# Token mix of a Fourier mixer on one core: order of GpSimd's sums, PE's chunk as one loop, first pairs among the last tiles of the MLP stage

## The chip, the cores and the metric

One core of a Trainium2 chip runs the whole program. The metric is the device time of the program in microseconds, lower is better. Several runs of each kernel are timed; one more execution is profiled, and every duration below comes from that one.

## The reference

Three blocks one after the other on x of 4 x 4224 x 192 in float32. The first is a causal convolution over 7 tokens whose weights are a softmax of `weight_gen`; the second adds the real part of a two-dimensional Fourier transform and an MLP. The third is the one that matters here:

```python
theta = x @ w_theta
zr, zi = x * np.cos(theta), x * np.sin(theta)
y = np.einsum('ts,bsd->btd', w_tok_r, zr) + np.einsum('ts,bsd->btd', w_tok_i, zi)
u = x + y
return u + np.maximum(u @ w_ch, 0.0)
```

The two einsums multiply weights of 4224 x 4224 with operands of 4224 x 768. They are the largest part of the work: the token mix.

## The kernel before, in words

**Stages.** A (convolution and the first Fourier pass), B (second Fourier pass), C (MLP, `run_c(step_c, ...)` over tiles n = 0 to 32 of 128 tokens, with the angle theta, its sine and cosine and z = x cos, x sin trailing a tile or two behind), M (token mix) and E (the last chunk of the mix, with the final product with `w_ch` woven in). Each engine has its own program; they meet only at semaphores.

**The token mix.** The tokens that are summed over are split into 11 chunks of three tiles. In each chunk 16 pairs of output tiles are treated, in four rounds `jj` of four pairs `i4` (pair p = 4 jj + i4), and a 33rd tile that is left over. A pair is a two by two block product (two output tiles, real and imaginary operand, two halves of the columns) done with seven products in place of eight, from sums and differences of blocks. A product is nine matmuls of 128x128 by 128x384 (three tiles, and each factor as a high and a low float32r part, without low by low), so a pair is 63 matmuls (`products`, L1448; `product`, L1456).

**Weights.** SP loads four blocks of a pair (`load_pair`, L463) into one of two buffers. GpSimd makes four sums of them (`sum_w`, L989, called by `sums`, L1029, which waits until the low parts of the pair before are made, because the four `wsum` tiles are single). ScalarE rounds each to its high part `wh` (`high_w`, L1154), VectorE subtracts for the low part `wl` (`low_w`, L720). The weights of pair p + 1 are made product by product while TensorE works on pair p.

**Operands.** The high and low parts of z for a chunk, `zh` and `zl`, stand twice, one set by `par`. While chunk c is multiplied, the three tiles of chunk c + 1 are prepared, one in each of the rounds jj = 0, 1, 2: SP loads the tile (`load_z`, L471) in the first pair of the round, GpSimd makes four sums (`sum_z`, L978), ScalarE and VectorE make seven high and low parts at the places of `ZPLACE` (L327): three in the second pair of the round (after products 1, 3 and 5), two in the third (after 2 and 5) and two in the fourth.

**Results.** After each product VectorE adds PSUM to the buffer `rbuf` of the pair (`add_r`, L778). In VectorE's program each `add_r(i)` is followed by `low_w` of the next pair and, where ZPLACE says so, by `low_z`. TensorE's product 2 waits for the add of product 0, product 4 for that of 2, product 6 for that of 4 (L1462 to L1469). So a VectorE instruction that waits holds back the adds that stand behind it, and with them TensorE.

**Loops.** TensorE's chunk (L1499) is a loop over three rounds, then the fourth round written out, then `left_m`. Chunks 1 to 8 are a loop of four passes over two chunks each (L1520). `chunk` of VectorE and ScalarE are built in the same way, as are their loops over two chunks (L860, L1254); the change leaves those loops as they are.

**The passage from C to M.** SP's order at the end of C: three loads of `rbuf`, `step_c` of NT, NT + 1 and NT + 2 (which store the last x2 and z tiles), a wait for all stores, the load of `rl`, and only then its M loop, whose first step loads weights for pair 2 and the z tile 3 (L502 to L536). VectorE reduces the last angles (`reduce_angle`, L710: four instructions on 128x768) between the first pairs' work (L838 to L857), ScalarE takes sines there (L1235 to L1252), GpSimd multiplies z (L1006, L1007) and rounds the turns (L1009, L1011) in its `step_c`. In the last tile of C, ScalarE's copy of theta (L1143) waits for the first instruction of `reduce_angle`, and TensorE's second half of `mlp_down` waits for that copy (L1443).

Of the kernel before, what the change touches and what calls it, by code (L numbers as in the profile page):

```python
# [31 lines left out]
ds = bass.ds  # L32
# [5 lines left out]
NT = S // P  # L38
# [4 lines left out]
NG = NT // 3  # L43
# [62 lines left out]
def token_fourier_mixer(nc, x_pad, wgen, f_seq, f_chan, f_rest, f_low, ident, w1, w2, w_theta, w_pairs, w_left,  # L106
# [15 lines left out]
    with ExitStack() as top:  # L122
# [160 lines left out]
        def live(m):  # L283
            return not isinstance(m, int) or 0 <= m < NT
# [19 lines left out]
        def flat(t):  # L304
            return t[:].rearrange("p b d -> p (b d)")
# [68 lines left out]
        def _(sp):  # L374
# [128 lines left out]
            sp.wait_ge(y_ready, 2 * NT)  # L503
            for k in range(3):
                load_r(k, k)
            for n in range(NT, NT + 3):
                step_c(n, n)
            sp.wait_ge(z_out, 16 * NT)
            sp.wait_ge(y_out, 16 * NT)
            sp.dma_start(flat(rl), y_scr[NT - 1:NT].rearrange("o p x -> p (o x)")).then_inc(rl_in, 16)  # L510


            def step_m(c, jj, i4):

                p = pair(jj, i4)
                last = isinstance(jj, int) and jj == 3
                sp.wait_ge(wl_ready, unit(c, p, 6))
                load_pair(i4 % 2, NPAIR * c + p + 2)
                if last and not i4:
                    load_left(c)  # L520
                if not last and not i4:
                    sp.wait_ge(zlo_ready, STEPS * (3 * (c + 1) + jj))
                    load_z(3 * (c + 1) + jj)
                sp.wait_ge(r_done, mixed(c, p, 6) + 2)
                sp.dma_start(y_scr[ds(2 * p, 2)].rearrange("i p x -> p i x"),
                             rbuf[i4][:].rearrange("p i b d -> p i (b d)")).then_inc(r_out[i4], 16)
                sp.wait_ge(r_out[(i4 + 3) % 4], 16 * (4 * c + jj + 1))
                load_r((i4 + 3) % 4, p + 3 if not last else (p + 3) % NPAIR)

            sp.sem_inc(r_out[3], 16)  # L530
            with sp.Fori(0, NG - 1) as c:
                with sp.Fori(0, 3) as jj:
                    for i4 in range(4):
                        step_m(c, jj, i4)
                for i4 in range(4):
                    step_m(c, 3, i4)  # L536


            LAST = NG - 1
# [48 lines left out]
        def _(dve):  # L588
# [142 lines left out]
            def step_c(n, s):  # L731
# [27 lines left out]
                    dve.tensor_tensor(ul2[:], bank[1][:], f32(uh2[:]), ALU.subtract).then_inc(ul_ready, 1)  # L759
                if preparing(n):  # L760
                    low_z(n - (NT - 3), 0, n - (NT - 3), HB)
                if live(n - 2):
                    reduce_angle(n)
                if isinstance(n, int) and n == NT - 1:
                    for i in range(3):
                        low_w(0, 0, i, 0)
                if live(n):
                    add_x2(n, s, 0)
                if live(n + 2):
# [74 lines left out]
            add_r(0, 0, 0, 0)  # L844
            low_w(0, 0, 5, 0)
            low_w(0, 0, 6, 0)
            reduce_angle(NT)
            low_w(0, 1, 0, 1)
            for i in range(1, 4):
                add_r(0, 0, 0, i)  # L850
                low_w(0, 1, i, 1)
            reduce_angle(NT + 1)
            for i in range(4, STEPS):
                add_r(0, 0, 0, i)
                low_w(0, 1, i, 1)
            for i4 in range(1, 4):
                step_m(0, 0, i4, 1)  # L857
            dve.wait_ge(rl_in, 16)
# [94 lines left out]
        def _(pool):  # L953
# [80 lines left out]
            def chunk(c, first=0):  # L1034
                with pool.Fori(first, 3) as jj:
                    for i4 in range(4):
                        sums(c, jj, i4)
                        if not i4:
                            sum_z(3 * (c + 1) + jj)
                for i4 in range(4):  # L1040
                    sums(c, 3, i4)
# [3 lines left out]
            pool.wait_ge(ut_ready, NT)  # L1045
            sum_w(0)
            step_c(NT, NT)
            step_c(NT + 1, NT + 1)
            sums(0, 0, 0)
            step_c(NT + 2, NT + 2)  # L1050
            sum_z(3)
            for i4 in range(1, 4):
                sums(0, 0, i4)
            chunk(0, 1)
            with pool.Fori(1, NG - 1) as c:
# [9 lines left out]
        def _(act):  # L1065
# [70 lines left out]
            def keep_x2(s):  # L1136
                act.activation(tile(s - 1)[:], x2s[:, :, 0:D], ACT.Copy).then_inc(x2_kept, 1)
# [32 lines left out]
            def step_c(n, s):  # L1170
# [18 lines left out]
                    high_z(n - (NT - 3), 0, n - (NT - 3), HB)  # L1189
                if live(n - 1):  # L1190
                    keep_x2(s)
                    keep_theta(n)
                if live(n - 2):
                    sines(n)
                if isinstance(n, int) and n == NT - 1:
                    act.wait_ge(hp_ready, HB * NT)
                    for i in range(3):
                        high_w(0, 0, 0, 0, i)

            def next_w(c, jj, i4, i):  # L1200

# [39 lines left out]
            act.wait_ge(y_ready, 2 * NT)  # L1241
            high_w(0, 0, 0, 0, 6)
            keep_x2(NT)
            keep_theta(NT)
            sines(NT)
            for i in range(4):
                next_w(0, 0, 0, i)
            sines(NT + 1)
            for i in range(4, STEPS):
                next_w(0, 0, 0, i)  # L1250
            for i4 in range(1, 4):
                step_m(0, 0, i4, 1)  # L1252
            chunk(0, 0, 1)
            with act.Fori(0, (NG - 3) // 2) as c2:  # L1254
# [59 lines left out]
        def _(pe):  # L1314
# [182 lines left out]
                    left(c, i, par)  # L1497

            def chunk(c, par, first=0):  # L1499
                with pe.Fori(first, 3) as jj:  # L1500
                    for i4 in range(4):
                        step_m(c, jj, i4, par)
                for i4 in range(4):
                    step_m(c, 3, i4, par)
                left_m(c, par)

            run_c(step_c, pe)
# [113 lines left out]
```

## Time and profile before

| | us |
|---|---|
| median of 3 runs | 3403.27 (3394.12 to 3410.21) |
| the profiled execution, its own time | 3414.97 |
| its span, first to last instruction | 3412.8 |
| TensorE busy with matmuls | 3026.9 (89%) |
| VectorE busy | 2680.5 (79%) |
| GpSimd busy | 1538.7 (45%) |
| ScalarE busy | 1244.2 (36%) |
| mean granted TensorE clock | 0.948 of full speed |
| one GpSimd sum on 128x384, means of the four kinds | 1.02 to 1.21 |
| store of a z tile, issue to landing, median | 3.4 |
| weights of a pair and a z tile, issue to landing, medians | 6.7 and 7.4 |

The span is cut into 40 slices on the profile's page; the token mix with its last chunk begins in the fourteenth (1136.8 us) and ends with the program. There the digits of TensorE are 9 with few exceptions. A matmul's busy time (334 ns) overlaps the next one's, since they start 173.5 ns apart, so the busy share hides losses under 0.2 us and says nothing of a slower clock; distances between starts do. PEldq, DVEq and SPq are the sequencers of TensorE, VectorE and SP.

### The profile page before, as it was taken

The page shows a single profiled execution, that of the slowest core. Times are in us where ns is not written, and L with a number is a line of the kernel's source. Part 1 is how long each engine was busy: PE and PEld are TensorE (multiplying, and loading weights), DVE is VectorE, ACT ScalarE, POOL GpSimd, SP SyncE. Part 2 cuts the span into 40 slices and gives each one's busy share as a digit, 9 for nine tenths or more (in the row PEclk, how much of TensorE's full clock was granted, in tenths as well). Part 3 has the DMA queues.
Part 4 walks back from the last instruction along what each step waited for, and adds up shares of the span by engine and source line. Part 5 has one row for each costly group of instructions (what it writes and reads, how often), then busy time and mean ns, then how long its engine had stood idle before and what let it go on. Part 6 is the DMA issues. An engine that isn't in the chain of part 4 may idle for free.

```text
span 3412.8 us, 57572 instructions
## 1 busy us (share of the span) xinstructions
PE 3026.9 (89%) x17218; PEld 2867.3 (84%) x17218; DVE 2680.5 (79%) x4407; ACT 1244.2 (36%) x2320; POOL 1538.7 (45%) x1494
## 2 busy tenths in 40 slices
PE   3555659999999599999989999899999999999999
PEld 2444328888888599999989999899999999999999
DVE  9999457999999577787767787677768788877776
ACT  1111224555555333333323333333333333333443
POOL 5676104666666444444434344344444444443221
PEclk8777889999999899999999999999999999999999
DMA  6655552233233356565556555555555556555432
GB/s 207 215 189 194 173 210 79 105 106 110 100 116 112 137 185 227 199 222 213 203 182 228 206 209 216 186 203 209 212 209 203 208 212 223 214 212 191 137 137 83
DMA packets 212275, 612.84 MB, mean 180 GB/s; under 512 B 15824, under 2 KB 59152, under 8 KB 212080
## 3 DMA queue, kind: packets, MB, share of 16 engines
q1 hardware_dynamic: 202928, 597.41, 49.1%
q10 hardware_dynamic: 9152, 12.98, 1.4%
q8 instruction: 104, 1.70, 0.2%
q14 instruction: 91, 0.75, 0.1%
HBM read 393.66 MB, written 216.66 MB: 179 GB/s over the span
## 4 chain that ended last, share of the span: by engine, by line
PE 60%; DVE 9%; issue 8%; POOLq 8%; DMA 6%; DVEq 3%; ACT 2%; POOL 2%; SPq 2%; ACTq 1%
PE banks L1452 48%; PE banks L1319 7%; POOLq L960 5%; DMA zraw<-z_scr 4%; DVE un L773 3%; DVE zl L728 2%; DVE angle L716 1%; PE banks L1380 1%; DMA fraw<-f_low 1%; POOLq L993 1%; DVEq L698 1%; DVEq L715 1%; POOL head L958 1%; PE banks L1533 1%; PE banks L1394 1%
## 5 line engine op out<-in xcount | busy, mean ns | idle before, releaser
L1452 PE MATMUL banks<-zh,wh 128*128 128x384 f32 x3828 | 1310.1, 342 | 107.6 <-DVE rbuf L785 91.4
L1452 PE MATMUL banks<-zl,wh 128*128 128x384 f32 x3828 | 1298.4, 339 | 10.9 <-issue 10.9
L1452 PE MATMUL banks<-zh,wl 128*128 128x384 f32 x3828 | 1299.0, 339 | 0.0
L785 DVE TENSOR_TENSOR rbuf<-rbuf,banks 128x384 f32<-128x384 f32 x1168 | 644.1, 551 | 309.0 <-PE banks L1452 281.9
L1452 PEld LDWEIGHTS banks<-zh,wh 128*128 128x128 f32 x3828 | 733.9, 192 | 121.0 <-DVE rbuf L785 61.8
L1452 PEld LDWEIGHTS banks<-zh,wl 128*128 128x128 f32 x3828 | 732.8, 191 | 11.4 <-issue 11.4
L1452 PEld LDWEIGHTS banks<-zl,wh 128*128 128x128 f32 x3828 | 733.9, 192 | 0.0
L1160 ACT ACTIVATE wh<-wsum 128x384 fp32r<-128x384 f32 x704 | 370.2, 526 | 883.5 <-PE banks L1452 758.9
L992 POOL TENSOR_TENSOR wsum<-wraw 128x384 f32<-128x384 f32 x176 | 179.4, 1019 | 1096.5 <-DVE wl L723 971.0
L723 DVE TENSOR_TENSOR wl<-wsum,wh 128x384 fp32r<-128x384 f32 x664 | 522.3, 787 | 96.8 <-ACT wh L1160 71.3
L1160 ACT ACTIVATE wh<-wraw 128x384 fp32r<-128x384 f32 x528 | 278.0, 526 | 490.3 <-PE banks L1452 476.8
L723 DVE TENSOR_TENSOR wl<-wraw,wh 128x384 fp32r<-128x384 f32 x498 | 302.8, 608 | 29.5 <-ACT wh L1160 21.1
L958 POOL TENSOR_TENSOR head<-head,tap 128x1152 f32<-128x1152 f32 x88 | 231.4, 2630 | 117.4 <-DVE tap L624 104.5
L1330 PE MATMUL banks<-fs,x1s 128*128 128x128 f32 x396 | 90.1, 422 | 182.2 <-DVE x1s L660 182.2
L1330 PEld LDWEIGHTS banks<-fs,x1s 128*128 128x128 f32 x396 | 84.3, 325 | 188.4 <-DVE x1s L660 159.6
L994 POOL TENSOR_TENSOR wsum<-wsum,wraw 128x384 f32<-128x384 f32 x176 | 212.1, 1205 | 28.0 <-issue 28.0
L997 POOL TENSOR_TENSOR wsum<-wraw,wsum 128x384 f32<-128x384 f32 x176 | 199.0, 1131 | 28.0 <-issue 28.0
L995 POOL TENSOR_TENSOR wsum<-wraw 128x384 f32<-128x384 f32 x176 | 186.9, 1062 | 0.0
L624 DVE TENSOR_TENSOR tap<-xin,banks 128x1152 f32<-128x1152 f32 x132 | 175.7, 1346 | 0.2
L1174 ACT ACTIVATE hh<-banks 128x512 fp32r<-128x512 f32 x198 | 118.2, 597 | 138.1 <-PE banks L1319 137.6
L1394 PE MATMUL banks<-w2s,hh 128*128 128x384 f32 x792 | 163.7, 341 | 5.3 <-DVE hl L703 4.2
L703 DVE SCALAR_TENSOR_TENSOR hl<-banks,hh 128x512 fp32r<-128x512 f32 x198 | 135.8, 686 | 21.1 <-ACT hh L1174 20.8
(140 smaller groups left out, 4218.7 us busy)
## 6 DMA issues: line engine op xcount, KB each, us to landing
wraw<-w_pairs SPq DMA_DIRECT2D x176, 768.0 KB, 6.7
rbuf<-y_scr SPq DMA_DIRECT2D x176, 768.0 KB, 5.7
y_scr<-rbuf SPq DMA_DIRECT2D x160, 768.0 KB, 4.0
xin<-x_pad SPq DMA_DIRECT2D x22, 1728.0 KB, 8.8
z_scr<-zsc SPq DMA_DIRECT2D x33, 768.0 KB, 3.4
zraw<-z_scr SPq DMA_DIRECT2D x33, 768.0 KB, 7.4
x_scr<-x1s SPq DMA_DIRECT2D x22, 576.0 KB, 5.3
t_scr<-tst ACTq DMA_DIRECT2D x44, 288.0 KB, 4.1
```

Of the source, the lines that this page charges most:

```text
L624: return dve.tensor_tensor(four(dst), tap_x(h, k), tap_w(h, k), ALU.mult)
L723: dve.tensor_tensor(wl[i][:], weights_of(k, i), f32(wh[i][:]), ALU.subtract).then_inc(wl_ready, 1)
L785: dve.tensor_tensor(part, part, dst(k, i), ALU.add).then_inc(r_done, 1)
L958: last = pool.tensor_tensor(head[h][:], head[h][:], tap[k - 1][:], ALU.add)
L992: pool.tensor_tensor(wsum[0][:], w21, w22, ALU.add).then_inc(s_sum, 1)
L994: pool.tensor_tensor(wsum[1][:], wsum[0][:], w11, ALU.subtract).then_inc(s_sum, 1)
L995: pool.tensor_tensor(wsum[2][:], w11, w21, ALU.subtract).then_inc(s_sum, 1)
L997: pool.tensor_tensor(wsum[3][:], w12, wsum[1][:], ALU.subtract).then_inc(s_sum, 1)
L1160: act.activation(wh[i][:], weights_of(k, i), ACT.Copy).then_inc(wh_ready, 1)
L1319: last = pe.matmul(dst, l, r, start=(t == 0), stop=(t == len(products) - 1))
L1394: pe.matmul(bank[4 + b][:, 0:2 * D], hh[:, k, P * b:P * b + P], w2s[:, k], start=(k == 0), stop=False)
L1452: last = pe.matmul(dst, l[w][:, q, :], r[par][:, operand, q, :], start=starts and q == 0 and t == 0, stop=q == 2 and t == 2, skip_group_ch ...
```

## The change

- GpSimd: in each round `sum_z` comes after the sums of the second pair, no longer after those of the first. At the start of M the sums for pair 1 come before `step_c(NT + 1)`, those for pair 2 after `step_c(NT + 2)` and before `sum_z(3)`.
- TensorE: a chunk is one loop over four rounds, then `left_m`.
- VectorE and ScalarE: in the last tile of C the first three weight parts of pair 0 come before `reduce_angle` and before `keep_theta` and `sines`. In the first pairs of M the last angles, sines and copies are spread anew. ScalarE's wait for all z and y stores, before it writes `zh` of the other set, stands after the first product of pair 1.
- SP: the loads for pair 2 (weights), of z tile 3 and of `rbuf` 3 are issued before the last z tiles are stored; stores and loads of the first two pairs stand between `step_c` of NT, NT + 1 and NT + 2; the load of `rl` comes later.

```diff
--- before.py
+++ after.py
@@ -503,12 +503,10 @@
             sp.wait_ge(y_ready, 2 * NT)
             for k in range(3):
                 load_r(k, k)
-            for n in range(NT, NT + 3):
-                step_c(n, n)
-            sp.wait_ge(z_out, 16 * NT)
-            sp.wait_ge(y_out, 16 * NT)
-            sp.dma_start(flat(rl), y_scr[NT - 1:NT].rearrange("o p x -> p (o x)")).then_inc(rl_in, 16)
-
+
+            def store_r(k, p):
+                sp.dma_start(y_scr[ds(2 * p, 2)].rearrange("i p x -> p i x"),
+                             rbuf[k][:].rearrange("p i b d -> p i (b d)")).then_inc(r_out[k], 16)
 
             def step_m(c, jj, i4):
 
@@ -522,18 +520,40 @@
                     sp.wait_ge(zlo_ready, STEPS * (3 * (c + 1) + jj))
                     load_z(3 * (c + 1) + jj)
                 sp.wait_ge(r_done, mixed(c, p, 6) + 2)
-                sp.dma_start(y_scr[ds(2 * p, 2)].rearrange("i p x -> p i x"),
-                             rbuf[i4][:].rearrange("p i b d -> p i (b d)")).then_inc(r_out[i4], 16)
+                store_r(i4, p)
                 sp.wait_ge(r_out[(i4 + 3) % 4], 16 * (4 * c + jj + 1))
                 load_r((i4 + 3) % 4, p + 3 if not last else (p + 3) % NPAIR)
 
-            sp.sem_inc(r_out[3], 16)
-            with sp.Fori(0, NG - 1) as c:
-                with sp.Fori(0, 3) as jj:
+            def chunk(c, first=0):
+                with sp.Fori(first, 3) as jj:
                     for i4 in range(4):
                         step_m(c, jj, i4)
                 for i4 in range(4):
                     step_m(c, 3, i4)
+
+            step_c(NT, NT)
+            load_r(3, 3)
+            load_z(3)
+            sp.wait_ge(wl_ready, unit(0, 0, 6))
+            load_pair(0, 2)
+            step_c(NT + 1, NT + 1)
+            sp.wait_ge(r_done, mixed(0, 0, 6) + 2)
+            store_r(0, 0)
+            sp.wait_ge(wl_ready, unit(0, 1, 6))
+            load_pair(1, 3)
+            step_c(NT + 2, NT + 2)
+            sp.wait_ge(r_out[0], 16)
+            load_r(0, 4)
+            sp.wait_ge(y_out, 16 * NT)
+            sp.dma_start(flat(rl), y_scr[NT - 1:NT].rearrange("o p x -> p (o x)")).then_inc(rl_in, 16)
+            sp.wait_ge(r_done, mixed(0, 1, 6) + 2)
+            store_r(1, 1)
+            sp.sem_inc(r_out[3], 16)
+            for i4 in range(2, 4):
+                step_m(0, 0, i4)
+            chunk(0, 1)
+            with sp.Fori(1, NG - 1) as c:
+                chunk(c)
 
 
             LAST = NG - 1
@@ -759,11 +779,11 @@
                     dve.tensor_tensor(ul2[:], bank[1][:], f32(uh2[:]), ALU.subtract).then_inc(ul_ready, 1)
                 if preparing(n):
                     low_z(n - (NT - 3), 0, n - (NT - 3), HB)
-                if live(n - 2):
-                    reduce_angle(n)
                 if isinstance(n, int) and n == NT - 1:
                     for i in range(3):
                         low_w(0, 0, i, 0)
+                if live(n - 2):
+                    reduce_angle(n)
                 if live(n):
                     add_x2(n, s, 0)
                 if live(n + 2):
@@ -844,15 +864,16 @@
             add_r(0, 0, 0, 0)
             low_w(0, 0, 5, 0)
             low_w(0, 0, 6, 0)
+            add_r(0, 0, 0, 1)
+            low_w(0, 1, 0, 1)
             reduce_angle(NT)
-            low_w(0, 1, 0, 1)
-            for i in range(1, 4):
+            for i in range(2, 6):
                 add_r(0, 0, 0, i)
-                low_w(0, 1, i, 1)
+                low_w(0, 1, i - 1, 1)
             reduce_angle(NT + 1)
-            for i in range(4, STEPS):
-                add_r(0, 0, 0, i)
-                low_w(0, 1, i, 1)
+            add_r(0, 0, 0, 6)
+            low_w(0, 1, 5, 1)
+            low_w(0, 1, 6, 1)
             for i4 in range(1, 4):
                 step_m(0, 0, i4, 1)
             dve.wait_ge(rl_in, 16)
@@ -1035,7 +1056,7 @@
                 with pool.Fori(first, 3) as jj:
                     for i4 in range(4):
                         sums(c, jj, i4)
-                        if not i4:
+                        if i4 == 1:
                             sum_z(3 * (c + 1) + jj)
                 for i4 in range(4):
                     sums(c, 3, i4)
@@ -1045,11 +1066,12 @@
             pool.wait_ge(ut_ready, NT)
             sum_w(0)
             step_c(NT, NT)
+            sums(0, 0, 0)
             step_c(NT + 1, NT + 1)
-            sums(0, 0, 0)
             step_c(NT + 2, NT + 2)
+            sums(0, 0, 1)
             sum_z(3)
-            for i4 in range(1, 4):
+            for i4 in range(2, 4):
                 sums(0, 0, i4)
             chunk(0, 1)
             with pool.Fori(1, NG - 1) as c:
@@ -1189,13 +1211,14 @@
                     high_z(n - (NT - 3), 0, n - (NT - 3), HB)
                 if live(n - 1):
                     keep_x2(s)
-                    keep_theta(n)
-                if live(n - 2):
-                    sines(n)
                 if isinstance(n, int) and n == NT - 1:
                     act.wait_ge(hp_ready, HB * NT)
                     for i in range(3):
                         high_w(0, 0, 0, 0, i)
+                if live(n - 1):
+                    keep_theta(n)
+                if live(n - 2):
+                    sines(n)
 
             def next_w(c, jj, i4, i):
 
@@ -1241,14 +1264,25 @@
             act.wait_ge(y_ready, 2 * NT)
             high_w(0, 0, 0, 0, 6)
             keep_x2(NT)
+            next_w(0, 0, 0, 0)
             keep_theta(NT)
+            next_w(0, 0, 0, 1)
+            next_w(0, 0, 0, 2)
             sines(NT)
-            for i in range(4):
-                next_w(0, 0, 0, i)
+            next_w(0, 0, 0, 3)
+            next_w(0, 0, 0, 4)
             sines(NT + 1)
-            for i in range(4, STEPS):
-                next_w(0, 0, 0, i)
-            for i4 in range(1, 4):
+            next_w(0, 0, 0, 5)
+            next_w(0, 0, 0, 6)
+            next_w(0, 0, 1, 0)
+
+            act.wait_ge(z_out, 16 * NT)
+            act.wait_ge(y_out, 16 * NT)
+            for i in range(1, STEPS):
+                next_w(0, 0, 1, i)
+                if i in ZPLACE[1]:
+                    high_z(3, 1, 0, ZPLACE[1][i])
+            for i4 in range(2, 4):
                 step_m(0, 0, i4, 1)
             chunk(0, 0, 1)
             with act.Fori(0, (NG - 3) // 2) as c2:
@@ -1497,11 +1531,9 @@
                     left(c, i, par)
 
             def chunk(c, par, first=0):
-                with pe.Fori(first, 3) as jj:
+                with pe.Fori(first, 4) as jj:
                     for i4 in range(4):
                         step_m(c, jj, i4, par)
-                for i4 in range(4):
-                    step_m(c, 3, i4, par)
                 left_m(c, par)
 
             run_c(step_c, pe)
```

## Rows read from the trace of the kernel before

**Rows 1.** The page, costliest group: busy us, mean ns | idle before it, releaser.

```profile
L1452 PE MATMUL banks<-zh,wh 128*128 128x384 f32 x3828 | 1310.1, 342 | 107.6 <-DVE rbuf L785 91.4
```

**Rows 2.** Waits, 1206 to 3124 us: us in total, times, longest.

```profile
POOL tbuf L982 <- DMA zraw<-z_scr: 122.5, 29, 5.8
...
PE banks L1452 <- DVE rbuf L785: 58.5, 29, 3.2
...
PE banks L1452 <- issue: 23.1, 6, 4.7
```

**Rows 3.** L1452 by stretch: us, PE (x), PEld (x), PEclk, DMA share, GB/s.

```profile
1228.30:1239.20 10.90, 10.90 (x65) 10.90 (x64) 1.00 0.79 290
1239.20:1254.60 15.40, 12.71 (x65) 12.42 (x64) 0.89 0.42 153
1385.50:1397.20 11.70, 11.22 (x65) 10.90 (x64) 1.00 0.57 204
1749.50:1778.40 28.90, 20.68 (x101) 20.17 (x101) 0.82 0.35 113
2143.60:2171.90 28.30, 20.00 (x100) 19.49 (x100) 0.82 0.35 115
2538.30:2564.40 26.10, 19.50 (x102) 19.04 (x101) 0.87 0.36 125
1206.50:3124.70 1918.20, 1836.61 (x10315) 1824.90 (x10315) 0.97 0.58 210
```

**Rows 4.** Timeline, one stall of pair 5: start us, us, instruction, [idle before].

```profile
1240.83 0.33 PE L1452 MATMUL banks<-zh,wh 128*128 128x384 f32 x1
...
1243.89 1.01 POOL L992 TENSOR_TENSOR wsum<-wraw 128x384 f32<-128x384 f32 x1
...
1244.93 0.53 ACT L1160 ACTIVATE wh<-wsum 128x384 fp32r<-128x384 f32 x1 [3.29 <-POOL wsum L992]
...
1247.67 0.54 DVE L785 TENSOR_TENSOR rbuf<-rbuf,banks 128x384 f32<-128x384 f32 x1
...
1245.34 0.34 PE L1452 MATMUL banks<-zh,wl 128*128 128x384 f32 x1
1248.36 0.41 PE L1452 MATMUL banks<-zh,wh 128*128 128x384 f32 x1 [2.69 <-DVE rbuf L785]
```

**Rows 5.** Timeline of VectorE, pair 1 of chunk 1, GpSimd busy until 1392.7.

```profile
1389.65 0.91 DVE L723 TENSOR_TENSOR wl<-wsum,wh 128x384 fp32r<-128x384 f32 x1
1390.48 1.36 DVE L728 TENSOR_TENSOR zl<-zraw,zh 128x384 f32 x1
...
1393.77 0.55 DVE L723 TENSOR_TENSOR wl<-wraw,wh 128x384 fp32r<-128x384 f32 x1
```

**Rows 6.** Sequencers around 1755 us: ns min/median/max, first and last start.

```profile
L1520 PEldq COMPARE_BRANCH  x1: 7207/7207/7207, 1752.8 to 1752.8; - x1
...
L860 DVEq MOVE  x1: 43/43/43, 1760.6 to 1760.6; - x1
```

**Rows 7.** Queue 8 by stretch, packets, MB: 1754 to 2149, then 3187 to 3256.

```profile
q8 instruction: 12, 0.20, 0.2%
...
q8 instruction: 4, 0.07, 0.5%
```

**Rows 8.** Timeline and waits of the passage into the token mix.

```profile
1128.35 0.81 ACT L1143 ACTIVATE theta<-banks 128x768 f32<-128x768 f32 x1 [4.83 <-DVE angle L713]
...
1134.71 1.92 DVE L723 TENSOR_TENSOR wl<-wraw,wh 128x384 fp32r<-128x384 f32 x1 [3.06 <-ACT wh L1160]
...
1141.45 0.56 DVE L699 TENSOR_TENSOR x2s<-x2s,banks 128x384 f32<-128x384 f32 x1
...
1174.49 2.14 POOL L1007 TENSOR_TENSOR zsc<-UR,zsc 128x768 f32<-128x768 f32 x1
1190.68 0.99 POOL L982 TENSOR_TENSOR tbuf<-zraw 128x384 f32<-128x384 f32 x1 [14.05 <-DMA zraw<-z_scr]
...
1199.34 0.66 PE L1452 MATMUL banks<-zh,wh 128*128 128x384 f32 x1 [17.36 <-DVE rbuf L785]
```

## The prediction

> **What bounds the kernel now.** I read the page first: matmuls fill 89% of the span, and the costliest group, the first matmul of a product, has idle time before it that VectorE's adds end [rows 1]. So TensorE bounds the token mix, and what can be won is its idle time and its slow clock. The waits of the stretch from pair 2 of the first chunk to the start of the last chunk come next [rows 2]: 29 waits for an add, 58.5 us in all, and 23.1 us that no semaphore explains ("issue").
>
> The view by stretches prices them [rows 3]. An undisturbed pair of 63 matmuls lasts 10.9 us (0.1735 us from start to start: 26 steps from 1240.83 to 1245.34 [rows 4]). The whole stretch of 1918.2 us holds 10315 of them, 1789.7 us at that rate, so 128.5 us are lost. Three places lose 11.7, 11.1 and 8.9 us, where 99 matmuls should last 17.2: the stretches at 1749.5, 2143.6 and 2538.3, at the turns of the loop over two chunks. That is 31.7. The other 97 are lost in 29 pairs, the second pair of each round with z work, 3.3 us each: twenty like the one of 15.4 us, and nine, in the first round of a chunk, like the one of 11.7.
>
> The timeline shows one [rows 4]. GpSimd waits in `sum_z` for the tile to land [rows 2], finishes it, and starts the weight sums at 1243.89, though their weights had long been there. ScalarE's `wh` waited 3.29 us for them, VectorE stood in `low_w` behind it, its add ran at 1247.67 and TensorE resumed at 1248.36 after 2.69 us. The other 1.7 us of the 4.5 are clock: the pair has a granted mean of 0.89 where its neighbour has 1.00 [rows 3].
>
> **Term 1, GpSimd's order.** Nothing is added; four operations of about 1.1 us (the table above) move behind four others. The weight sums now start when the low parts of the pair are done, 1.4 us into the second pair (as in every other pair), so the 3.29 us wait goes. `sum_z` follows at +6.2 and ends at about +11; its consumers, the parts of number 3 on, come after product 2 of the third pair, at +15.6. No wait takes its place there, and the tile has landed. What is late next is VectorE. The pair has 7 adds, 7 `low_w` and 3 `low_z`. Beside GpSimd a `low_w` took 0.91 and a `low_z` 1.36 us; after GpSimd stopped, 0.55 [rows 5]. Adds read PSUM and took 0.54. Now GpSimd works through all of the second pair. By hand, from the pair's start: add 0 at 1.9, `low_w` 0 uncontended to 3.0, add 1 at 3.4, `low_w` 1 to 5.1, `low_z` to 6.4, add 2 to 7.0, but TensorE wanted it at 6.24: 0.8 us lost. This is what pair 1 of a chunk shows today, where sums and `sum_z` also adjoin: 11.7 us [rows 3]. Then `low_w` 2 to 7.9, add 3, `low_w` 3 to 9.2, `low_z` to 10.3, add 4 to 10.8: TensorE waits 0.7 us more before product 6. I take 1.5 us a pair, 43.5 in all, and no slow clock, since the 11.7 us pair kept 1.00 [rows 3]. Gain 97 - 43.5, about 54. Bounds: 0.7 a pair as in the first rounds (gain 77); or 2.9 us, when each stall passes 1 us and the clock drops as well (gain 13).
>
> **Term 2, TensorE's loop.** It takes 252 matmuls with their weight loads out of each chunk's code and adds a branch per chunk and register arithmetic for four pairs. The turns of the round loop cost nothing that shows: a pair after one lasts 10.9 us [rows 3], so I cost the new turn at 0; its cover is the queue of matmuls already issued. The outer turns are different: the branch of L1520 took 7.2 us, and a second hole of 4 us followed [rows 6]. Each pass over two chunks fetched 12 blocks of 16 KB on queue 8 [rows 7]. In the last chunk a loop over four pairs, 476 matmuls and as many weight loads, fetched 4 in its first pass and none in the second, so the engine keeps at least that many, and a block holds about 952 / 4 = 238 of these instructions. The body of the outer loop is 2 x 540 matmuls today, 2160 / 238 = 9.1 blocks, and 2 x 288 afterwards, 4.8. Between 4 (kept) and 9 (not kept) nothing is measured; 4.8 is near 4, so I take kept. The Trainium skill ("Runtime: NRT & Kernel Launch", Instruction fetch mechanics) gives TensorE 128 KiB, eight such blocks; by that a jump back of five, with two fetched ahead, just fits. The same section says that a taken branch outside the current two pages forces a fetch; by that rule every turn, the round loop's of two blocks and more included, should stall, and term 2 would be 0. The second pass without a fetch speaks against it here.
>
> With TensorE's branch gone, VectorE's is late next: after its own branch it went on only at 1760.6 [rows 6], unseen beside TensorE's 7.2 us. Its first add would come at about 1761.1, TensorE wants it at 1758.9. With the add, about 2.9 us of stall and 1.7 of clock stay: 4.6 each. Gain 31.7 - 14 = 18. Bounds: 0 and 31.
>
> **Term 3, the passage into M.** Today: two `reduce_angle`, two rounds of sines, the z products until 1176.6 [rows 8], their store, `rl`, then weights and z tile 3 in SP's order, so that `sum_z` starts at 1190.68 (14.05 us of wait), the sums for pair 2 after it, and TensorE resumes at 1199.34 after 17.36. The steps afterwards, each with the durations of the same operations:
> - Three `low_w` before `reduce_angle`: about 3.3 us against GpSimd's operations. The copy of theta, today 1128.35 to 1129.16, ends at 1131.9. The last four `mlp_down` groups wait for it: 2.7 us **lost**, TensorE's last MLP matmul at 1135.7.
> - But the 5 us of `low_w` from 1134.71 are out of the way of the second x2 sum, today ready at 1142.0: now 1137.0. Product 2 runs at 1142.7, the parts of pair 0 are ready at 1143.7, and SP sends for the weights of pair 2 then, having sent for z tile 3 before. GpSimd's sums for pair 1 run from 1143.8. Product 4 of pair 0 starts at 1151.4.
> - The angles remain a chain: sines to 1153.4, z products and turns to 1159.2, last angle 1162.8, sines 1165.5, z products 1169.5 (today 1176.6), store landed 3.4 us later, 1173. ScalarE waits for that store in the middle of pair 1, and everything behind it waits too: its parts for pair 2, VectorE's `low_w` and adds. Then `wh` 1173.7, `low_w`, `low_z`, add: TensorE at 1176 where it was 1199.34. Gain 1199.3 - 1176 = **23**. The store of z tile 32, the weights for pair 2 and 3 and z tile 3 are then no longer in a row: that is where the time comes from. SP's longer waits (for pair 0's adds before `store_r`) hold only the load of `rbuf` 0 for pair 4, three pairs ahead.
> Bounds: only SP's order helps (gain 10); no contention for `low_w` and angles (32).
>
> **Sum.** 54 + 18 + 23 = 95 us off the profiled execution's 3414.97, so 3320. The median of the timed runs is 11.7 lower, 3403.27, and the same 95 off it give **3308**.
>
> **Rivals.**
> 1. *Only the first stall of a pair remains*, 0.7 us: term 1 gives 77, the time is 3285. For: pair 1 today. Against: there GpSimd stopped after the first `low_z`. Chance 0.12.
> 2. *The outer turn still misses*: the engine keeps four blocks and not 4.8, so term 2 is 0 and the time 3403 - 54 - 23 = 3326. For: only four are shown [rows 7]. Against: the distance is small beside the 9.1 that is known to be too far. The two-page rule cited above from the Trainium skill would give the same time. Chance 0.18.
> 3. *Contention is dearer*: 2.9 us a pair with slow clock; 3403 - 13 - 18 - 23 = 3349. Chance 0.10.
> 4. *Slower*: VectorE's ten operations on two SBUF tiles each wait for a whole GpSimd operation, 1.36 us [rows 5], in every second pair. 13.6 + 7 x 0.55 = 17.5 us against 10.9, 6.6 lost x 29 = 191; 3403 + 191 - 97 - 41 = 3456. It decides from 4.8 us a pair ((97 + 41) / 29). Against: GpSimd has eight operations there, so at most eight such waits, which is just 4.9. Chance 0.05.
> 5. *The change does not do what it says*: another wait ends where `wh` waited (`low_z` work moves along, the weights' load), the loss of 3.3 a pair stays and term 3 is eaten by its 2.7 and the late store; within 0.5%, 3400. Against: the 3.29 us wait names GpSimd alone [rows 4]. Chance 0.05.
>
> **Numbers.** The forecast has 0.50. A measurement tells about 0.5%, 17 us, from no change; the forecast and rivals 1 to 3 lie beyond it: faster 0.90, same 0.05, slower 0.05. The forecast's own range is 3290 to 3335. The range wanted reaches over the rivals 1 to 3, with the dearest combination left out: 3268 to 3360.
>
> **What would show it.** Right: no wait of ScalarE for the first weight sum in rounds with z work; GpSimd's wait for z tiles near 0; second pairs of 12.4 us at a clock of 1.00; a mean of `low_w` on sums above today's; queue 8 with some 55 to 60 packets for 104 and no branch of 7 us; the 17.36 us wait gone and the first chunk 23 us shorter. Wrong: second pairs over 14 us, or a stall at each turn of TensorE's round loop, or the last half of `mlp_down` later by more than 3 us.

## The result, and the profile after

The changed kernel takes 3319.16 us (median, 3315.71 to 3320.27); beside it the kernel before took 3402.22 us. The ratio is 0.9754, 95% interval 0.973 to 0.9779: 83 us less, where 95 had been forecast (3308) within a range of 3268 to 3360. The profiled execution took 3315.71 us, 99.3 less than that of the kernel before.

The page of the changed kernel. Line numbers have moved: L1486 is the matmul that was L1452, L805 the add that was L785.

```profile
span 3313.6 us, 57585 instructions
...
q8 instruction: 59, 0.97, 0.1%
...
L1486 PE MATMUL banks<-zh,wh 128*128 128x384 f32 x3828 | 1296.1, 339 | 58.1 <-DVE rbuf L805 58.1
```

Idle time before the first matmul of a product fell from 107.6 [rows 1] to 58.1 us, and the part that no semaphore explained is gone from the line. Queue 8 carried 59 packets of 16 KB in place of 104; 55 to 60 had been forecast.

The same stretches as in [rows 3]: an undisturbed pair, pair 1 of chunk 1, the three turns of the loop over two chunks, and everything from pair 2 to the last chunk.

```profile
1189.10:1200.00 10.90, 10.90 (x65) 10.90 (x64) 1.00 0.61 218
...
1352.00:1364.60 12.60, 11.52 (x65) 10.88 (x64) 1.00 0.51 190
1706.80:1727.80 21.00, 19.09 (x101) 18.77 (x101) 0.92 0.44 152
2082.70:2102.30 19.60, 17.52 (x101) 17.20 (x101) 1.00 0.48 163
2457.20:2478.30 21.10, 19.08 (x100) 18.76 (x100) 0.92 0.44 151
1178.40:3025.50 1847.10, 1809.43 (x10316) 1789.01 (x10316) 1.00 0.60 217
```

The last row is to be held against 1918.2 us in [rows 3]: 71.1 us of the gain are here, at a mean clock of 1.00 where it was 0.97. A turn takes 19.6 to 21.1 us where it took 26.1 to 28.9; 17.2 would be undisturbed. Every second pair of a round with z work, 29 of them, now takes 12.6 us. That is less than the 15.4 of the second and third rounds, and more than the 11.7 of the first.

The waits in that stretch, us in total, times, longest:

```profile
PE banks L1486 <- DVE rbuf L805: 37.7, 61, 2.1
...
ACT wh L1182 <- POOL wsum L1016: 20.1, 21, 1.0
```

TensorE's waits for adds are twice as many and shorter (61 against 29, 37.7 us in all against 58.5 [rows 2]). GpSimd's wait for the z tile, 122.5 us before, is no longer in the list, nor is ScalarE's wait for the first weight sum, the 3.29 us of [rows 4]. One second pair, VectorE first and then GpSimd (start us, us, instruction, idle before):

```profile
2106.32 1.21 DVE L743 TENSOR_TENSOR wl<-wsum,wh 128x384 fp32r<-128x384 f32 x1 [0.15 <-ACT wh L1182]
2107.45 1.37 DVE L748 TENSOR_TENSOR zl<-zraw,zh 128x384 f32 x1
2108.74 0.54 DVE L805 TENSOR_TENSOR rbuf<-rbuf,banks 128x384 f32<-128x384 f32 x1
...
2111.31 1.37 DVE L748 TENSOR_TENSOR zl<-zraw,zh 128x384 f32 x1
2112.60 0.54 DVE L805 TENSOR_TENSOR rbuf<-rbuf,banks 128x384 f32<-128x384 f32 x1
...
2103.69 1.01 POOL L1013 TENSOR_TENSOR wsum<-wraw 128x384 f32<-128x384 f32 x1 [8.98 <-DVE wl L743]
...
2107.27 1.13 POOL L1018 TENSOR_TENSOR wsum<-wraw,wsum 128x384 f32<-128x384 f32 x1 [0.16 <-issue]
2108.37 1.31 POOL L1003 TENSOR_TENSOR tbuf<-zraw 128x384 f32<-128x384 f32 x1
...
2112.42 1.12 POOL L1008 TENSOR_TENSOR tbuf<-zraw,tbuf 128x384 f32<-128x384 f32 x1 [0.16 <-issue]
```

GpSimd starts the weight sums when the parts of the pair are done and works on until 2113.5. Beside it a `low_z` took 1.37 us, twice, each right before an add that TensorE waited for. TensorE resumed at:

```profile
2109.34 0.44 PE L1486 MATMUL banks<-zh,wh 128*128 128x384 f32 x1 [0.64 <-DVE rbuf L805]
2113.20 0.44 PE L1486 MATMUL banks<-zh,wh 128*128 128x384 f32 x1 [0.47 <-DVE rbuf L805]
```

These are products 4 and 6, the two places that the prediction named. The Trainium skill ("SBUF — State Buffer", SBUF: two separate sides) says that VectorE with two SBUF inputs and GpSimd share a port pair that one of them holds for a whole instruction. The rows agree: at 2107.45 `low_z` has a GpSimd operation ahead of it until 2108.40 and ends 0.42 us after that one, while adds, which read one operand from PSUM, took 0.54.

The passage into the token mix. The first row is the start of the last tile's `mlp_down`, the second that of its other half, then two waits in pair 1:

```profile
1116.37 0.44 PE L1428 MATMUL banks<-w2s,hh 128*128 128x384 f32 x1 [1.21 <-DVE hl L723]
...
1123.07 0.44 PE L1428 MATMUL banks<-w2s,hh 128*128 128x384 f32 x1 [3.02 <-ACT theta L1165]
...
1162.00 0.66 PE L1486 MATMUL banks<-zh,wh 128*128 128x384 f32 x1 [11.49 <-DVE rbuf L805]
1171.65 0.66 PE L1486 MATMUL banks<-zh,wh 128*128 128x384 f32 x1 [4.53 <-DVE rbuf L805]
```

From the first of these to pair 2 (1178.41) it is 62.0 us. In the kernel before it was 81.8: 1124.73 to 1206.51, the second being 1199.34 [rows 8] and the rest of pair 1. So 19.7 us of the gain are here. The wait of 17.36 us is gone; the two of 11.49 and 4.53 us above are what is left.

**The account.** 71.1 + 19.7 = 90.8 of the 99.2 us between the two spans. The other 8.4 lie ahead of the last MLP tile (1124.73 against 1116.37), in code that is the same: over twelve profiled executions, this pair and the ten below, that point lay between 1116.4 and 1125.4 us. It is scatter that this pair of profiled executions happened to have in favour of the change.

### The profile page after: what moved, and what is told of

Read it like the earlier page. It is cut to its first block, busy times and chain, and to the rows that moved or that the text cites. A ratio compares the mean times of both kernels' runs of the same rounds, so it can differ in the third digit from the quotient of the medians.

```text
span 3313.6 us, 57585 instructions
## 1 busy us (share of the span) xinstructions
PE 2993.9 (90%) x17218; PEld 2826.7 (85%) x17218; DVE 2691.4 (81%) x4407; ACT 1245.2 (38%) x2320; POOL 1549.1 (47%) x1494
## 4 chain that ended last, share of the span: by engine, by line
PE 66%; DVE 11%; issue 8%; POOLq 6%; DVEq 3%; DMA 2%; ACT 2%; POOL 1%; ACTq 1%; SPq 0%
PE banks L1486 54%; PE banks L1353 7%; POOLq L981 5%; DVE un L793 3%; DVE zl L748 2%; DVE angle L736 2%; DVE wl L743 1%; PE banks L1414 1%; DMA fraw<-f_low 1%; DVEq L735 1%; DVEq L718 1%; POOL head L979 1%; PE banks L1565 1%; DVE angle L733 1%; PE banks L1428 1%
## 5 line engine op out<-in xcount | busy, mean ns | idle before, releaser
L1486 PE MATMUL banks<-zh,wh 128*128 128x384 f32 x3828 | 1296.1, 339 | 58.1 <-DVE rbuf L805 58.1
L1486 PE MATMUL banks<-zh,wl 128*128 128x384 f32 x3828 | 1283.3, 335 | 0.0
L1486 PE MATMUL banks<-zl,wh 128*128 128x384 f32 x3828 | 1282.8, 335 | 0.0
L805 DVE TENSOR_TENSOR rbuf<-rbuf,banks 128x384 f32<-128x384 f32 x1168 | 643.0, 551 | 271.5 <-PE banks L1486 235.7
L1486 PEld LDWEIGHTS banks<-zh,wh 128*128 128x128 f32 x3828 | 721.2, 188 | 79.8 <-DVE rbuf L805 53.5
L1486 PEld LDWEIGHTS banks<-zl,wh 128*128 128x128 f32 x3828 | 721.4, 188 | 0.0
L1486 PEld LDWEIGHTS banks<-zh,wl 128*128 128x128 f32 x3828 | 720.9, 188 | 0.0
L1013 POOL TENSOR_TENSOR wsum<-wraw 128x384 f32<-128x384 f32 x176 | 179.0, 1017 | 1139.9 <-DVE wl L743 1014.5
L743 DVE TENSOR_TENSOR wl<-wsum,wh 128x384 fp32r<-128x384 f32 x664 | 535.4, 806 | 44.9 <-ACT wh L1182 23.4
L743 DVE TENSOR_TENSOR wl<-wraw,wh 128x384 fp32r<-128x384 f32 x498 | 287.4, 577 | 13.6 <-ACT wh L1182 4.6
L1016 POOL TENSOR_TENSOR wsum<-wraw 128x384 f32<-128x384 f32 x176 | 178.7, 1015 | 0.0
L723 DVE SCALAR_TENSOR_TENSOR hl<-banks,hh 128x512 fp32r<-128x512 f32 x198 | 135.7, 685 | 19.7 <-ACT hh L1196 19.2
```

Source lines behind the costliest of these rows:

```text
L743: dve.tensor_tensor(wl[i][:], weights_of(k, i), f32(wh[i][:]), ALU.subtract).then_inc(wl_ready, 1)
L805: dve.tensor_tensor(part, part, dst(k, i), ALU.add).then_inc(r_done, 1)
L1013: pool.tensor_tensor(wsum[0][:], w21, w22, ALU.add).then_inc(s_sum, 1)
L1016: pool.tensor_tensor(wsum[2][:], w11, w21, ALU.subtract).then_inc(s_sum, 1)
L1486: last = pe.matmul(dst, l[w][:, q, :], r[par][:, operand, q, :], start=starts and q == 0 and t == 0, stop=q == 2 and t == 2, skip_group_ch ...
```

## The experiments

Each ran with the kernel before on the same chip, whose median was 3415 us beside terms 1, 2 and 3 undone and the z parts moved, 3416 beside the short z sums and the turns written out, and 3425 beside the other four. The changed kernel itself was run once more, as one of those four. So what follows is compared with 3319 to 3324 us and, more sharply, in the trace. "The stretch" is always pair 2 of the first chunk to the last chunk, 10315 matmuls or so (1847.1 us in the changed kernel), "the passage" the last tile's first `mlp_down` matmul to pair 2 (62.0 us).

**The changed kernel again.** No edit.

> The changed kernel itself, beside the others on one chip, since the runs of the kernel before on the chip of the first experiments had a median of 3415 and not 3402. Expected: 3319 within 5 us; the parts undone singly (48 to 58, 22 and 21 us above it) should then add up to the distance to the kernel before.

Measured: 3324.46 us, ratio 0.9709 (0.9678 to 0.974); stretch 1848.7, passage 65.4 us. Beside its own runs of the kernel before the gain is 101 us by medians. The first comparison gave 83 us, and the two intervals overlap only between 0.973 and 0.974. So timing the whole program gives the gain of the change no better than to some 20 us; the trace's 91 lie between. The passage alone differs by 3.4 us between two executions of this one kernel.

**Term 1 undone.**

```diff
-                        if i4 == 1:
+                        if not i4:
                             sum_z(3 * (c + 1) + jj)
```

> The changed kernel with one part undone: in each round GpSimd makes the z sums after the weight sums of the first pair again. Theory (term 1): the second pair of a round goes back from 12.6 to about 15 us in rounds 1 and 2 of a chunk and to about 11.6 in round 0, 97 us lost in 29 pairs in place of 29 x 1.7 = 49, so 48 us more than the changed kernel: 3367. Rival: the order only moves GpSimd's work about and the gain came from the other parts: within 17 us of the changed kernel's 3319.

Measured: 3377.76 us, 53 to 59 above the changed kernel, somewhat more than expected. The stretch:

```profile
1186.90:3089.60 1902.70, 1832.14 (x10316) 1820.94 (x10316) 0.98 0.59 211
```

It is 55.6 us longer. The 29 second pairs alone lose 59 us more than in the changed kernel; the turns lose 3 less, since TensorE's clock fell at none of them. The waits of [rows 2] are back, and dearer than they were:

```profile
POOL tbuf L1003 <- DMA zraw<-z_scr: 127.7, 29, 5.6
ACT wh L1182 <- POOL wsum L1013: 80.4, 24, 4.4
PE banks L1486 <- DVE rbuf L805: 70.5, 29, 3.8
```

Nothing but the order of GpSimd's sums in the rounds differs, so this order is the largest part of the change.

**Term 2 undone.**

```diff
-                with pe.Fori(first, 4) as jj:
+                with pe.Fori(first, 3) as jj:
                     for i4 in range(4):
                         step_m(c, jj, i4, par)
+                for i4 in range(4):
+                    step_m(c, 3, i4, par)
                 left_m(c, par)
```

> The changed kernel with TensorE's fourth round written out again. Theory (term 2): the loop over two chunks is 9.1 blocks of code again, its three turns cost 31.7 us in place of the 10 that the changed kernel's trace shows, so 22 us more: 3341, with a branch of 5 to 7 us at each turn and about 100 fetches on queue 8. Rival: VectorE's late turn costs as much whatever TensorE does: the time stays at 3319, though the branch is long.

Measured: 3341.47 us, 17 to 22 above the changed kernel, 22 expected; the stretch is 1867.4 us, 20.3 more. The branch at the turn (ns min/median/max) and the queue on the page:

```profile
L1554 PEldq COMPARE_BRANCH  x4: 67/6327/7250, 1712.2 to 2858.9; - x4
...
q8 instruction: 104, 1.70, 0.2%
```

Three long branches as in [rows 6] (the short one is the loop's end), while the branch in the kernel with term 1 undone, which has the loop over four rounds, takes 209 ns at most. The rival falls: VectorE's late turn alone costs less.

**How much code is kept.** The fourth round is written out in one chunk of the two (`pe.Fori(first, 3 if par else 4)`, and the round after it only `if par`).

> The changed kernel with TensorE's fourth round written out in one of the two chunks of a pass only: 2 x 828 instructions, 7.0 blocks by 238 a block, between the 4.8 that were kept and the 9.1 that were not. Theory of a store of eight blocks of which two are fetched ahead and five lie behind: a jump back of seven misses, branches of 5 to 7 us at the three turns, 20 us more than the changed kernel: 3339. Rival: seven blocks are still kept: no difference.

Measured: 3333.65 us, 9 to 14 above the changed kernel; the stretch is 1862.5 us, 15.4 longer. Both are less than the 20 expected. The jump back misses:

```profile
L1555 PEldq COMPARE_BRANCH  x4: 67/5532/5848, 1718.5 to 2860.4; - x4
...
q8 instruction: 90, 1.47, 0.2%
```

By the forecast's estimate of 238 instructions a block, 7.0 blocks are too many and 4.8 are few enough. Where between them the limit lies stays open; it agrees with the forecast's picture of eight blocks, two fetched ahead and five behind, without proving it.

**Term 3 undone.** The kernel before with the two edits of terms 1 and 2 alone.

> The kernel before with the two steady parts of the change alone (order of GpSimd's sums in the rounds, TensorE's loop over four rounds); the passage from the MLP stage into the token mix is as before. Theory (term 3): the passage is worth 20 us, so 3339. Rival: the passage is worth nothing on the clock, since what it wins is lost in the last MLP tile and in later waits: 3319.

Measured: 3340.24 us, 16 to 21 above the changed kernel; passage 83.1 us (1120.19 to 1203.25) and stretch 1847.2, the changed kernel's. TensorE's waits from the last MLP tile to pair 2 are those of the kernel before again:

```profile
PE banks L1452 <- DVE rbuf L785: 33.6, 6, 17.0
PE banks L1452 <- DVE wl L723: 3.9, 1, 3.9
```

**One part of term 3: the order in the last MLP tile.**

```diff
+                if live(n - 2):
+                    reduce_angle(n)
                 if isinstance(n, int) and n == NT - 1:
                     for i in range(3):
                         low_w(0, 0, i, 0)
-                if live(n - 2):
-                    reduce_angle(n)
```

and in ScalarE's program `keep_theta` and `sines` again ahead of the three `high_w`.

> The changed kernel with the order in the last tile of the MLP stage undone: VectorE reduces the angle before the first three low weight parts, ScalarE copies theta and takes the sines before the three high parts. Theory: the 2.7 us that TensorE's last mlp_down groups now wait come back, but the second x2 sum, pair 0 and the chain of angles start 5 us later: 2 to 5 us slower than the changed kernel. Rival: this part only costs its 2.7 us and the kernel is that much faster without it. Too little for the clock; the trace decides, by the start of pair 2 counted from the last MLP tile.

Measured: 3329.59 us against 3324.46, and a passage of 69.5 us (1125.39 to 1194.91) against 62.0 and 65.4. The wait of `mlp_down` for theta shrinks from 3.02 to 0.8 us, and what it bought comes back:

```profile
PE banks L1486 <- DVE wl L743: 3.9, 1, 3.9
PE banks L1414 <- DVE x2s L719: 2.9, 1, 2.9
PE banks L1428 <- DVE hl L723: 1.3, 1, 1.3
PE banks L1428 <- ACT theta L1165: 0.8, 1, 0.8
```

In the changed kernel the order pays 2.2 us there and saves 4 to 7.5 us of the passage net. The times agree, 5 us apart, as far as they can tell so little.

**The contention by itself.** GpSimd's z sums of the rounds are made on 32 of their 384 columns (`sum_z(3 * (c + 1) + jj, 32)`).

> The changed kernel with GpSimd's z sums of the rounds made on 32 of 384 columns; the other columns of the sums keep what an earlier tile left, so the operands made from them are not the reference's. All else is as in the changed kernel. Theory: of the two stalls of a second pair, the one before product 4 (0.81 us) comes from low_z beside the weight sums and stays, the one before product 6 (0.61, with what follows 0.9) comes from low_z beside the z sums and goes: second pairs of 11.7 us, 29 x 0.9 = 26 us less than the changed kernel: 3294. Rival: contention doesn't matter, VectorE has too many instructions in that pair: 12.6 us stay.

Measured: 3297.46 us, 22 to 27 below the changed kernel. The stretch:

```profile
1182.10:3009.50 1827.40, 1802.27 (x10317) 1791.06 (x10316) 1.00 0.61 219
```

The 29 second pairs lose 27.1 us in place of 48.5: in the trace TensorE's hole before product 4 stands (0.98 us from start to start, 0.17 of it the matmul) and the one before product 6 is gone. In the same pair as above the first `low_z` still takes 1.37 us and the second 0.55. VectorE's program is unchanged, so what cost before product 6 are GpSimd's operations beside it, not the number of VectorE's own.

**The z parts moved.** This and the next two are no part of the change; they follow from the reading of the stalls.

```diff
-        ZPLACE = {1: {1: 0, 3: 1, 5: 2}, 2: {2: 3, 5: 4}, 3: {2: 5, 5: 6}}
+        ZPLACE = {1: {6: 0}, 2: {3: 1, 5: 2, 6: 3}, 3: {3: 4, 5: 5, 6: 6}}
```

> The changed kernel with the places of the z parts moved: one in the second pair of a round (after its last product), three in the third and three in the fourth (after products 3, 5, 6), in place of three, two, two. Theory: the 1.7 us that a second pair still loses are VectorE's low z parts beside eight operations of GpSimd; away from them nothing is lost in any pair, 29 x 1.7 = 49 us less than the changed kernel: 3270. Rival: VectorE is simply full in a pair with three low z parts, and the loss moves to the third and fourth pairs, twice 29 pairs: no faster than 3319, or slower.

Measured: 3272.38 us, ratio 0.9583 (0.9567 to 0.9599). The stretch:

```profile
1180.98:2979.30 1798.32, 1792.45 (x10315) 1790.45 (x10315) 1.00 0.62 223
```

It is 48.8 us shorter than the changed kernel's, 49 expected; every second, third and fourth pair of a round lasts 10.9 us, so the hole before product 4 is gone too. Three low z parts do fit into a pair where GpSimd is idle in its second half.

**ScalarE's wait later in the passage.** On top of the z parts moved:

```diff
-            act.wait_ge(z_out, 16 * NT)
-            act.wait_ge(y_out, 16 * NT)
             for i in range(1, STEPS):
                 next_w(0, 0, 1, i)
                 if i in ZPLACE[1]:
+                    act.wait_ge(z_out, 16 * NT)
+                    act.wait_ge(y_out, 16 * NT)
                     high_z(3, 1, 0, ZPLACE[1][i])
```

> The kernel with the z parts moved (3272 us) with one further edit: at the start of the token mix ScalarE waits for the stores of z and y only before its first z part, after product 6 of pair 1, in place of before the weights of product 1. Theory: the wait of 4.9 us of TensorE before product 4 of pair 1 goes, 5 us less: 3267. Rival: the wait for the store is only moved to product 6 and beyond and TensorE meets it there: 3272.

Measured: 3265.90 us, 6.5 less; the passage is 56.5 us, 5.4 less than with the z parts moved alone, where 5 had been expected. TensorE's waits for adds in it are 11.5 us and two short ones, 3.4 together, beside the 3.0 for theta; the one of 4.5 us before product 4 is gone. With the wait ahead of the weights' parts, ScalarE and everything queued behind it had stood still for a store that only the z parts need.

**VectorE's and ScalarE's turns written out.** On top of both:

```diff
-            with dve.Fori(0, (NG - 3) // 2) as c2:
+            for c2 in range((NG - 3) // 2):
```

and the same for ScalarE.

> The last kernel (z parts moved, late wait: 3266 us) with the loop over two chunks written out four times for VectorE and ScalarE; TensorE, GpSimd and SP keep their loops. Theory: what a turn still costs (2.2 to 3.9 us, three times) is that VectorE starts about 4 us late behind its own backward branch; with no branch a first pair lasts 10.9 us everywhere, 9 us less: 3257. Rival: it is TensorE's own branch or ScalarE's fetching that costs there, or the longer straight code makes new waits: no gain.

Measured: 3253.75 us, ratio 0.9527 (0.9512 to 0.9543), 12 us less. The stretch, 8.9 us shorter than 1796.8 us before this edit, 9 expected:

```profile
1176.30:2964.20 1787.90, 1787.90 (x10315) 1787.21 (x10314) 1.00 0.62 224
```

TensorE is busy for the whole of it. 1787.9 us for 10315 matmuls is 0.1733 each: nothing is left to win there but the matmuls themselves. Because VectorE's and ScalarE's loops were written out together, the run does not tell which of the two was late; the trace of the changed kernel names VectorE (term 2 below). This is the fastest kernel of the study, 65 to 71 us below the changed one.

## Why the prediction was right, and where it was off

| | forecast | trace, before against after | undone alone, in the trace |
|---|---|---|---|
| term 1, GpSimd's order | 54 | 98.2 - 48.5 = 49.7 | 55.6 |
| term 2, TensorE's loop | 18 | 31.7 - 10.1 = 21.6 | 20.3 |
| term 3, the passage | 23 | 81.8 - 62.0 = 19.7 (before rounding) | 21.1 |
| sum | 95 | 91.0 | 97.0 |

98.2 and 48.5 us are what the 29 second pairs last beyond 10.92 us each, 31.7 and 10.1 what the three turns last beyond 17.2. The mechanism of each term came as forecast. The sum is closer than its terms are: term 1 was 4 us too high, term 2 4 too low and term 3 3 too high, and that two of these errors cancelled is luck.

**Term 1.** The step by hand through the second pair held to a few tenths: losses before products 4 and 6, 0.81 and 0.61 us by the starts of the matmuls where 0.8 and 0.7 were forecast. The pair is 12.6 us and not 12.4, since the matmul after each hole is followed 0.28 us later by the next, not 0.17. 29 x 1.7 is about the 48.5 us left. A sign that had been named is there as well: `low_w` on sums takes 806 ns in the mean where it took 787. Rival 1 (only the first stall) is excluded: the second showed in all 29 pairs, and with GpSimd's z sums cut short it vanished. Rival 3's dearer contention did not come either; no hole reached 1 us of waiting, and the clock stayed at 1.00. Rival 4's slower outcome would have needed ten waits for whole GpSimd operations in a pair. In the pair shown VectorE had two of 1.37 and one of 1.21, and the rest between 0.55 and 0.89. Rival 5 (another wait takes the place of the old one) did not come: a pair loses 1.7 us and not 3.3.

**Term 2.** The outer loop's code was kept at 4.8 blocks, and rival 2 falls: TensorE's branch takes 0.21 us, and from 1713 to 2089 us, a whole pass, queue 8 carried no packet, where [rows 7] had 12. The reason why a turn still costs was named rightly: VectorE goes on late after its own branch. The sequencer of VectorE in the changed kernel:

```profile
L881 DVEq COMPARE_BRANCH  x1: 63/63/63, 1713.9 to 1713.9; - x1
L881 DVEq MOVE  x1: 43/43/43, 1717.1 to 1717.1; - x1
```

Its next instruction comes 3.2 us after the branch, where the kernel before had 3.9 (1756.7 to 1760.6 [rows 6]). The add that TensorE waited for started at 1717.68, with no wait on ScalarE in between, and TensorE resumed at 1718.29.

A turn lost 3.8, 2.4 and 3.9 us and not 4.6, and two things were off in that term. The waits were 2.1, 2.2 and 2.2 us, not 2.9. And the slow clock, put at 1.7 us for every turn, came at two of the three: the granted mean of the 4 us after the wait was 0.57 at the first turn and 1.00 at the second. The waits do not tell the two apart, so the 1.4 us that this gave are luck. That VectorE's wait after its branch is a fetch of code, as TensorE's long branch is taken to be, was not tested. It is hidden as long as TensorE's is longer.

**Term 3.** The forecast came out 3 us too high. The step that failed is the landing of the last z tile's store, put at 3.4 us. The chain of waits in the changed kernel, start, us, what:

```profile
1161.41 0.35 SPq L464
...
1161.81 7.01 DMA z_scr<-zsc
...
1168.84 0.53 ACT wh L1182
1169.37 0.02 issue
1169.39 1.17 DVE wl L743
```

The store took 7.01 us. The change puts the load of 768 KB of weights for pair 3 (L464) just ahead of it. The prediction had these transfers "no longer in a row", but only their order is reversed: it counted SP's waits and not what its transfers do to each other. All traces here agree: in the ten with this order, the load issued 0.4 us before, the store took 6.9 to 8.9 us, and in the two with the old passage, with no transfer issued in the 8 us before it, 3.39. This makes the load the likely cause; the order of the two was not tried by itself. A smaller part is that SP stood before the load, waiting for VectorE until 1161.4 us, while the z products had ended at 1161.0, so the store was issued 0.8 us after them. That SP's longer waits held nothing but the load of `rbuf` 0 is thus not quite so.

The cost in the last MLP tile was seen beforehand: 2.7 us by the prediction, 3.02 of wait in the trace, of which 0.8 was there before, so 2.2. That the copy of theta stands in front of `mlp_down` is nowhere in the diff and only in TensorE's program.

**The sum.** 91 to 97 us in the traces against 95 forecast, and 83 and 101 by the medians of two comparisons. The interval of the first comparison (2.2% to 2.7%, 75 to 92 us) does not reach the 95 that were forecast, and that of the second, 89 to 110 us, does. The kernel before scattered from 3394 to 3430 us over all its runs here, and the changed one from 3316 to 3325. By the trace, part of the scatter arises ahead of the last MLP tile. Why it is wider in the kernel before is not settled.

## What to carry to other kernels

Where an engine works through its program in order, put what waits for a transfer behind what has its data, and then ask which engine the moved work now stands beside: here the sums moved from a wait into contention, and 49 of the 98 us came back only when VectorE's parts were moved away too. TensorE's loop paid at each turn as long as its body was 7 blocks of code or more; a branch of several us and packets on the instruction queue show it. Shortening it brought the next engine's turn to light. A wait for a store belongs in front of the first instruction that needs it, not at the head of the block.

## What the runs showed of the hardware that was not expected

- TensorE's jump back over 7.0 blocks of 16 KB (by 238 instructions a block, an estimate from [rows 7]) cost a branch of 5.5 to 5.8 us, over 9.1 blocks 5.4 to 7.3, and over 4.8 at most 0.21. The Trainium skill ("Runtime: NRT & Kernel Launch", Instruction fetch mechanics) has a taken branch outside a window of two pages wait for a fetch. The loop over 4.8 blocks contradicts that, and so does the one over four blocks in [rows 7], whose second pass had no packet on queue 8.
- A store of 768 KB took 6.9 to 8.9 us, in ten traces, when a load of 768 KB was issued 0.4 us before it, and 3.4 in the two where none was issued in the 8 us before.
- Stalls of 0.5 to 0.9 us, two in a pair, left the granted clock at 1.00 in the stretches above; one of 2.69 us went with a mean of 0.89 for its pair [rows 3, 4]. The length does not decide by itself: after a hole of 2.91 us from start to start at 1626.36 us the kernel before kept 1.00, and so did the changed kernel at its second turn, with a wait as long as at the first, where the mean fell to 0.57.
- The same code up to the last MLP tile took between 1116.4 and 1125.4 us from one profiled execution to the next.
